# All six layer-2 tiles in pairs, with the weight sums made beside layer 1's last tile

## The reference

```
for t in range(768):                       # state per batch (4) and head (8), 48 x 48
    cur = einsum('bhd,bhe->bhde', u * k[t], v[t])
    y[t] = einsum('bhd,bhde->bhe', r[t], state + cur)
    state = w * state + einsum('bhd,bhe->bhde', k[t], v[t])
h = x @ w_in;  x = (h * sigmoid(1.702 * h)) @ w_out          # layer 1
h = x @ w_in2; out = (h * tanh(softplus(h))) @ w_out2        # layer 2
```

## Time and profile before

| | us |
|---|---|
| median of 3 runs | 878.36 |
| the profiled execution, its own time | 878.19 |
| its span, first to last instruction | 876.4 |
| PE busy | 869.5 |
| ACT busy | 345.1 |
| DVE busy | 330.9 |
| POOL busy | 216.6 |

### The profile page before, as it was taken

The page is one execution under the profiler, slowest core; times in us unless marked ns, Lnnn a source line. Parts: engine busy times, 40 slices in busy tenths (PEclk is TensorE's granted clock), DMA queues, the critical chain, the costliest instruction groups (busy, mean ns, idle before and its releaser), DMA issues.

```text
span 876.4 us, 13103 instructions
## 1 busy us (share of the span) xinstructions
PE 869.5 (99%) x5098; PEld 718.1 (82%) x5098; DVE 330.9 (38%) x501; ACT 345.1 (39%) x638; POOL 216.6 (25%) x200
## 2 busy tenths in 40 slices
PE   8999999999999999999999999999999999999998
PEld 7998888887888888778888888888888888888886
DVE  7756245424433442433254322211333333433333
ACT  4543232232223222322354532343544446544444
POOL 5869314222331432220000010173320003100000
PEclk9999999999999999999999999999999999999999
DMA  9454222312420422221431000110000000100001
GB/s 266 155 194 127 70 54 73 85 44 64 111 70 11 120 71 64 60 67 31 164 96 36 22 3 1 49 36 25 18 20 1 0 1 1 73 0 1 1 1 72
DMA packets 40432, 51.65 MB, mean 59 GB/s; under 512 B 6162, under 2 KB 32659, under 8 KB 40371
## 3 DMA queue, kind: packets, MB, share of 16 engines
q1 hardware_dynamic: 39840, 50.62, 19.8%
q10 hardware_dynamic: 530, 0.20, 0.1%
HBM read 38.21 MB, written 4.72 MB: 49 GB/s over the span
## 4 chain that ended last, share of the span: by engine, by line
PE 98%; DVE 1%; issue 0%; ACT 0%; POOL 0%; POOLq 0%; DVEq 0%; ACTq 0%
PE h L1352 31%; PE acc L1381 30%; PE h L1424 14%; PE acc L1520 7%; PE pair L1520 5%; PE a_bank L1231 3%; PE a_bank L1520 2%; PE pair L1264 2%; PE pair L1277 1%; PE a_bank L1289 1%; DVE wout_lo L1056 0%; PE pair L1214 0%; PE h L1231 0%; PE acc L1214 0%; DVE arena L1028 0%
## 5 line engine op out<-in xcount | busy, mean ns | idle before, releaser
L1352 PE MATMUL h<-xs,win_hi 128*128 128x512 f32 (+1 forms) x828 | 232.5, 380 | 0.9 <-DVE g_lo L1086 0.6
L1086 DVE TENSOR_TENSOR g_lo<-h,g_hi 128x512 fp32r<-128x512 f32 (+1 forms) x138 | 90.0, 652 | 332.1 <-ACT g_hi L767 332.1
L1352 PEld LDWEIGHTS h<-xs,win_hi 128*128 128x128 f32 x828 | 147.8, 188 | 31.2 <-issue 1.7
L763 ACT ACTIVATE h<-h 128x512 f32<-128x512 f32 (+1 forms) x138 | 76.2, 552 | 175.6 <-PE h L1352 172.7
L767 ACT ACTIVATE g_hi<-h 128x512 fp32r<-128x512 f32 (+1 forms) x138 | 78.3, 567 | 169.8 <-PE acc L1381 169.0
L1381 PE MATMUL acc<-g_hi,wout_hi 128*128 128x512 f32 (+1 forms) x414 | 112.6, 374 | 0.0
L1381 PE MATMUL acc<-g_hi,wout_lo 128*128 128x512 f32 (+1 forms) x414 | 112.4, 374 | 0.0
L1381 PE MATMUL acc<-g_lo,wout_hi 128*128 128x512 f32 (+1 forms) x414 | 112.4, 374 | 0.0
L1352 PE MATMUL h<-xs,win_lo 128*128 128x512 f32 (+1 forms) x414 | 110.4, 375 | 0.0
L577 POOL TENSOR_TENSOR arena<-arena 112x1024 f32<-112x1024 f32 x20 | 47.8, 2388 | 193.2 <-DMA arena<-in_rk 187.4
L1352 PEld LDWEIGHTS h<-xs,win_lo 128*128 128x128 f32 x414 | 75.0, 188 | 14.5
(11 more groups left out here) (154 smaller groups left out, 1117.1 us busy)
## 6 DMA issues: line engine op xcount, KB each, us to landing
arena<-in_rk SPq DMA_DIRECT2D x46, 192.0 KB, 3.4
mid<-in_wts SPq DMA_DIRECT2D x16, 384.0 KB, 7.3
arena<-in_wts SPq DMA_DIRECT2D x16, 384.0 KB, 3.4
xs<-xt SPq DMA_DIRECT2D x117, 48.0 KB, 2.0
arena<-in_k SPq DMA_DIRECT2D x22, 192.0 KB, 3.7
arena<-in_r SPq DMA_DIRECT2D x22, 192.0 KB, 4.0
arena<-in_v SPq DMA_DIRECT2D x22, 192.0 KB, 3.8
out<-mid SPq DMA_DIRECT2D x4, 768.0 KB, 3.3
```

The lines of the kernel that those rows point to most:

```text
L763: act.activation(h_cols(g), h_cols(g), GATES[layer]).then_inc(g_full, 1)
L1086: dve.tensor_tensor(g_lo[:, g % 2, cols], h_cols(g), f32(g_hi[:, g % 2, cols]), ALU.subtract).then_inc(glo_done, 1)
L1352: ins = pe.matmul(hb, w[:, f, kd, :], x_part(lo, par, kd)[:, c0:c1], start=i + kd == 0, stop=i == 2 and kd == KD - 1)
```

## The change

- Layer 2 has no plain tiles any more: TILES is 6 (layer 1 alone), PAIRS is 3. `split_mid` is gone, and `gate` serves layer 1 alone.
- The handover from tiles to quads now stands behind layer 1's last tile (tile 5), whose steps also split layer 2's weights.
- The weight sums are made from the staged weights in tile 5's steps, not from a reload. `stage` has four pieces: two in the area that later holds `h_sum`, `x_copy` and `seventh`, two in the place of tile 5's results in `mid`. A load into a piece waits for the low parts of the weight pair that used it too.
- The fourth weight sum is written over a raw block in its stage; its high and low parts always go to the place of feature block 0 of the odd hidden block, so odd w_in pieces are split for two of their three blocks.
- ScalarE does weight pair j in step 2j+2, the last in step 15; the table load moves to step 14. Factors B21 and B11 come in step 0, T2 and T3 in step 1, T4 in step 3, X20 in step 5.
- T4 and X20 change places in the order of factors, and `first_part` waits for X20 only ahead of its second product. The first pair's sums T2, T3, T4 lie in a free part of the arena, those of a later pair in the tile of `mid` before it.
- The split of w_out 15 goes into the first quad. The results of tile 5 are copied out when all weights are split.

```diff
-PLAIN = 2
-TILES = NT + PLAIN
-PAIRS = (NT - PLAIN) // 2
+TILES = NT
+PAIRS = NT // 2
-B21, B11, T2, T3, X20, T4, B22, X21, T1 = range(9)
+B21, B11, T2, T3, T4, X20, B22, X21, T1 = range(9)
...
-        STG = 8
-        stage = [arena[:, n * 2 * DM:(n + 1) * 2 * DM] for n in range(STG)]
+        shared = free(3 * TT, arena)
+        STG = 4
+        stage = [shared[:, 0:2 * DM], shared[:, 2 * DM:4 * DM]]
+        stage += [mid[:, (NT - 1) * KD * TT + n * 2 * DM:(NT - 1) * KD * TT + (n + 1) * 2 * DM] for n in range(2)]
...
         def raw_of(p, i):
-            t0 = PLAIN + 2 * p
+            t0 = 2 * p
             if i in (T2, T3, T4):
-                return mid_cols(0, (T2, T3, T4).index(i))
+                if p == 0:
+                    return t_first[:, 0:TT] if i == T2 else t_first[:, TT:2 * TT]
+                return mid_cols(t0 - 1, (T2, T3, T4).index(i))
...
         def fourth(j, lo):
-            return s4_more[:, lo] if j == FP - 1 else (win_hi, win_lo)[lo][:, 2 * j + 1, 0, :]
+            return (win_hi, win_lo)[lo][:, 2 * j + 1, 0, :]
...
 # SyncE, load_weights
                 if f >= STG:
                     sp.wait_ge(win_ready, NF + f - STG + 1)
                     sp.wait_ge(wout_ready, NF - 2 + f - STG + 1)
+                    sp.wait_ge(w_lo, 2 * ((f - STG) // 2 + 1))
...
 # GpSimd
             def weight_sums(j):
-                pool.wait_ge(w_raw_in[j % 2], 32 * (j // 2 + 1))
+                for f in (2 * j, 2 * j + 1):
+                    pool.wait_ge(stage_in[f % STG], 16 * (f // STG + 1))
                 if j:
                     pool.wait_ge(w_lo, 2 * j)
...
                 pool.wait_ge(w_sum, 4 * j + 3)
-                pool.tensor_tensor(w_sums[:, 3], raw[:, 0, 1], w_sums[:, 1], ALU.subtract).then_inc(w_sum, 1)
+                pool.wait_ge(win_ready, NF + 2 * j + 1)
+                pool.tensor_tensor(raw_in(j, 0, 1), raw_in(j, 0, 1), w_sums[:, 1], ALU.subtract).then_inc(w_sum, 1)
...
-            for i in (B21, B11):
-                factor_lo(0, i)
+            x_sums(0)
+            factor_lo(0, B21)
+            factor_lo(0, B11)
             weight_sums(0)
+            factor_lo(0, T2)
+            factor_lo(0, T3)
+            last_sum(0)
             for j in range(FP):
                 weight_lo(j)
                 if j + 1 < FP:
                     weight_sums(j + 1)
-                if j == 0:
-                    x_sums(0)
-                if j == 1:
-                    for i in (T2, T3, X20, T4):
-                        factor_lo(0, i)
+                if j < 2:
+                    factor_lo(0, (T4, X20)[j])
...
 # ScalarE
-            def tile(layer, par, t, last):
-                switch = layer == 0 and last
+            def tile(par, t, last):
                 for s, g in enumerate(range(BASE[t], BASE[t + 1])):
-                    if switch and g + 1 == BASE[t + 1]:
+                    if g + 1 < BASE[-1]:
+                        gate(g + 1)
+                    if g + 2 == BASE[-1]:
                         act.preload_act_table(GATES[1])
-                        gate(1, g + 1)
-                    elif g + 1 < BASE[-1]:
-                        gate(layer, g + 1)
...
-                    if switch:
+                    if last:
                         split_in(1, s)
                         if s >= 1:
                             split_out(1, s - 1)
...
+                        for i in {0: (B21, B11), 1: (T2, T3), 3: (T4,), 5: (X20,)}.get(s, ()):
+                            factor_hi(0, i)
+                        if s >= 2 and s % 2 == 0:
+                            weight_hi(s // 2 - 1)
+                        if s == NF - 1:
                             weight_hi(FP - 1)
...
             def quad(q):
                 if q == 0:
+                    split_out(1, NF - 1)
                     for i in (B22, X21, T1):
                         factor_hi(0, i)
...
 # TensorE
             def first_part(q):
                 j = q % FP
-                factors_there(q, X20 + 1)
+                if q < FP:
+                    pe.wait_ge(win_ready, NF + 2 * j + 2)
+                factors_there(q, B11 + 1)
...
                 product(x_bank, own(2 * j, 1), B21, True)
+                factors_there(q, X20 + 1)
                 product(x_bank, own(2 * j, 2), X20, False, True).then_inc(x_ready, 1)
```

More of the change, by code:

```diff
@@ L407, in mlp_rwkv_program, with run_tiles @@
         x_bank, sum_bank = h_bank[BASE[TILES] % 2], h_bank[(BASE[TILES] + 1) % 2]
[L409 to L412, removed]
+        def run_tiles(tile):
+            for t in range(TILES):
+                tile(t % 2, t, t == TILES - 1)
         @block.sync
@@ L507, in _ @@
                 load_weights(f)
[L509 to L526, removed]
             for p in range(PAIRS):
                 for i in range(2):
-                    t = PLAIN + 2 * p + i
+                    t = 2 * p + i
                     if t < NT - 2:
@@ L713, in _ @@
                 x_sums(p)
+                last_sum(p)
                 for i in range(FACTORS):
@@ L727, in split_in @@
                     raw = staged_in(f)
-                act.activation(win_hi[:, f], raw, ACT.Copy).then_inc(win_h, 1)
+                skip = layer and f % 2
+                act.activation(win_hi[:, f, skip:KD], raw[:, skip:KD], ACT.Copy).then_inc(win_h, 1)
             def split_out(layer, f):
@@ L767, in gate, with copy_out @@
                 act.activation(g_hi[:, g % 2, 0:c1 - c0], h_cols(g), ACT.Copy).then_inc(g_done, 1)
[L769 to L775, removed]
+            def copy_out(t, kds=BY_ACT):
+                layers = 2 if t == TILES - 1 else 1
+                act.wait_ge(win_ready, layers * NF)
+                act.wait_ge(wout_ready, layers * NF - 2)
+                if t == TILES - 1:
+                    act.wait_ge(w_lo, 2 * FP)
                 for kd in kds:
@@ L849, in tile @@
                             split_out(1, s - 1)
[L850 to L860 removed]
+                        for i in {0: (B21, B11), 1: (T2, T3), 3: (T4,), 5: (X20,)}.get(s, ()):
[3 more added lines that the diff above has]
+                        if s == NF - 1:
                             weight_hi(FP - 1)
[L862 to L863 removed]
+                if not last:
+                    copy_out(t)
             def weight_hi(j):
                 act.wait_ge(w_sum, 4 * (j + 1))
[L868 to L871 removed]
+                act.activation(s_hi[:, j], w_sums, ACT.Copy).then_inc(w_hi, 1)
+                act.wait_ge(h_done, BASE[TILES - 1] + 2 * j + 2)
+                act.activation(fourth(j, 0), stage[2 * j % STG][:, P:2 * P], ACT.Copy).then_inc(w_hi, 1)
             def factor_hi(p, i):
@@ L913, in pair_copy @@
             def pair_copy(p, i, kd):
-                act.wait_ge(f_lo, (p + 1) * FACTORS)
+                act.wait_ge(f_lo, (p + 1) * FACTORS + (T4 + 1 if i and p + 1 < PAIRS else 0))
                 if kd < KD - 1:
@@ L1140, in tile @@
                         decay_k(s // 7)
-                    if switch:
+                    if last:
                         split(s, s - 1 if s else None)
-                    if s == 1 and t == NT:
-                        split(None, NF - 1)
-                    if s in MID_STEPS and (layer == 1 and not last or switch):
-                        split_mid(1 - par, t + 1, MID_STEPS.index(s))
-                if t < TILES - 1:
-                    copy_out(layer, t)
+                if not last:
+                    copy_out(t)
             def pair_sum(n):
@@ L1189, in quad @@
                         pair_low(n + 1)
+                    if q == 0 and c == 0:
+                        split(None, NF - 1)
                     if q == 0 and c == 1:
-                        copy_out(1, TILES - 1)
+                        copy_out(TILES - 1)
                     if j == 0 and p and c < 2:
                         pair_copy(p - 1, c)
-            run_tiles(tile, 0)
-            run_tiles(tile, 1)
+            run_tiles(tile)
             for q in range(QUADS):
```

144 lines of the change are left out of this document (56 added, 88 removed).

## The result

The changed kernel took 879.67 us (median of 12 runs, 878.49 to 881.24), the kernel before 877.72 us beside it (12 runs, 877.25 to 878.95): a ratio of 1.0020, 95% interval 1.0011 to 1.0029. Measured once more in the first experiment, with runs of its own, the ratio was 1.0009 [0.9999, 1.0019]. The change buys nothing: by the first measurement it costs 2.0 us, by the second 0.8, which its interval does not tell from none.

A forecast was written before the change was run, and what follows sets the result against it. TensorE was taken to bound the kernel (busy 99%, 98% of the chain). From 878.36 us, -5.44 + 4.91 + 0.05 (one more split before the factors) + 0.8 = +0.3 gave 878.7 us; 8-in-10 range 877.0 to 882.3.

The forecast's parts named there:

- Matmuls removed: Layer 2's two plain tiles become a pair: 576 matmuls become 552, 24 fewer at 0.227 us, -5.44 us.
- The handover: From layer 1's last tile to the first quad: late weight results delay copy_x(0), so third(0) starts 4.9 us later.
- the lock: VectorE and GpSimd holding each other up when VectorE subtracts two SBUF tensors while GpSimd works; taken at +0.8 us.
- VectorE against GpSimd: In the handover's chain, two VectorE subtractions meet GpSimd's operations and one engine waits: +0.8 us, bounds 0 and 1.0.
- The upper bound: 1.0 us for VectorE and GpSimd contention, when each VectorE subtraction is let in between two GpSimd operations.
- The first rival: Slower: the idle gap before second(0) lowers TensorE's clock, +2.0 to +3.8 us, 880.7 to 882.5; chance 0.20.
- 21 matmuls, less 1.3 hidden: Upper clock price: second(0), third(0) and pair_down(0) all slow, +4.8 us, less 1.3 hidden in the second gap.
- Late loads: Layer 1's last tile: staging loads wait for weight sums with four stages; costed at nothing, 0 to 2 us each at worst.
- the order T4 then X20 at two boundaries: Pair boundaries: the second product waits for one more GpSimd operation, with 1.1 us of room; costed at nothing.
- The second rival: Slower: layer 1's last tile stalls on late loads or VectorE's queue, 879.5 to 882, most likely 880.7; chance 0.08.
- The rival on the other side: Faster: the last pair's weight results are done by 492.6, the handover's stall stays small, 872.9 us; chance 0.12.
- half way: The faster case with the handover's chain shorter by only 2 us: 876.5 us, sign turning from 1.5 us of shortening.

The follow-up runs named there:

- the first experiment: The changed kernel run again unaltered, beside the kernel before: 878.97 us against 878.22, ratio 1.0009.
- e4: Changed kernel with ScalarE's and VectorE's order in layer 1's last steps altered (sums 5 to 7 and w_in 14 earlier, table load last in step 14): 872.72 us.
- e6: Changed kernel with VectorE's subtractions for w_in 15 and w_out 14 moved from step 15 into the first quad: 879.45 us, ratio 1.0019.
- e2: Changed kernel with 16 spare matmuls on TensorE in the wait ahead of second(0): 878.45 us, ratio 0.9998.
- e5: Kernel before, with ten spare copies on ScalarE delaying copy_x(0): 884.43 us against 877.74, ratio 1.0076.
- e3: Changed kernel with the activation table load moved from step 14 to the end of step 15, behind the copy of sums 7: 877.36 us, ratio 0.9992.

## Why the prediction was right, point by point

The forecast was 878.7 us, "within 0.2%"; measured were 879.67 and, beside other runs, 878.97. As a difference from the kernel before, the forecast was +0.3 us, and +1.95 and +0.75 were measured. The starting value had luck in it: 878.36 was a median of three runs, 0.64 above that of twelve, and this brought the forecast nearer to the time that was measured.

- **Matmuls removed, -5.44.** Held. PE x5074, full windows in the quads, and e4 gets the whole of it.
- **The handover, +4.91.** Held. third(0) came 5.22 us later relative to first_part(0), of which 0.29 is the lock. Each link came at its length, from the table load to the 2.84 us (forecast 2.81) from the end of copy_x(0) to third(0).
- **VectorE against GpSimd, +0.8.** The mechanism was right, the size too large: 0.29 (e6). The upper bound had each of VectorE's two subtractions hold GpSimd up for its own 0.5 us. VectorE did most of the waiting (0.90 us for the one at 490.43, which takes 0.42 in e6's trace), and GpSimd lost only 0.18 and 0.11 us. The Trainium skill, SBUF — State Buffer, section Who interferes with whom, says that a VectorE instruction with two inputs in SBUF contends with a GpSimd instruction that reads SBUF. The rows agree (0.64 against 0.46 on GpSimd, 0.90 against 0.42 on VectorE); what it cost the chain was far less than the length of an operation.
- **The first rival, the clock.** I priced it as an alternative, and it came true together with the forecast. The Trainium skill, TensorE: Matmul & The Clock Gate, section HAM oscillation, says that idle gaps of TensorE can make the chip halve its clock. The trace agrees: a granted clock of 0.52 behind the gap. Its price was too high: 1.2 us (e2) instead of 2.0 to 3.8. The upper end was also added up wrongly: 4.8 less 1.3 is 3.5. The step that failed is "21 matmuls, less 1.3 hidden": the clock was back at 502.0, when third(0) ended, so pair_down(0)'s 9 matmuls never ran slowly. Of the 12 that did, six hid entirely in the second gap. In e5 the slow stretch lay later, nothing of it could hide, and it cost 2.6 us; which place it takes I could not have told from the profile of before.
- **Why the total fits.** In part by luck. The lock was 0.5 too dear and the clock, which the sum had at nothing, 1.2 too cheap: two errors of opposite sign. Of the sum of +0.3 the traces show +0.98 up to pair_down(0), and that is inside the forecast's own range. The rest of the 1.95 us between the first two medians, some 0.2 in the profiled span and what scatter adds, I didn't trace; the repeat gave 0.75.
- **Costed at nothing.** Late loads, VectorE's queue in the last tile, the order T4 then X20 at two boundaries: no wait of TensorE at any of them. The second rival didn't happen.
- **The rival on the other side** (weight results in time) didn't happen, but e4 shows that its arithmetic was right: 872.9 forecast for it, 872.72 measured once the order made it true. "Every link has a measured length" was the reason against it, and the links were only in that order because the kernel was written so. Two of its other figures don't follow from the sum: half way gives 878.7 - 2 = 876.7, not 876.5, and the sign of +0.3 turns with 0.3 us of shortening, not with 1.5.

## What to carry to other kernels

Before counting a saving on the bounding engine, follow the last result of the moved work through each queue it now stands in; if the order of three other engines was laid out for the old place, expect to need a new one, and here one that changed neither work nor buffers was worth 6 us. A new idle gap on TensorE can have a second price behind it: with 3.66 to 3.98 us in the profiles here the clock fell in nearly every run, with 2.91 in most. The price is smaller where the slow matmuls are followed by a wait for something else. A collision of two engines that exclude each other is worth looking up by who waits: here most of it fell on the one that wasn't on the chain.

## What the runs showed of the hardware

TensorE's granted clock fell to about half for a few microseconds after a gap in one place of a run that is otherwise full. With a gap of 3.98 us the whole run's clock was under 0.999 in all 23 runs of the changed kernel, with 3.68 us in nine of the ten of e6, with 3.66 us in all four of e5, with 2.91 in 7 of 10 (e3), and with 0.44 us or the gap filled in none. The gaps are those of the profiled run of each kernel; those of the other runs are not known. When it falls isn't fixed: the changed kernel's clock was already low when second(0) began, in e5 it fell some 1.4 us after second(0) had begun, and the cost behind the gap differed accordingly. In both profiled runs the slow stretch was some 7 us, an estimate from the windows (0.82 over the 4.1 us of the gap, if it is a step from 1.0 to 0.5, is a fall at about 495.1, and the clock is full again from 502.0; in e5, 0.67 over 2.5 us and 0.64 over the last 3 make it from about 628.3 to 635.2). It is not as long in every run: 8 of the 23 have a whole run's clock of 0.998 and not 0.996 or 0.997, which is 3 to 4 us at half the clock. For the first of these, the windows of the changed kernel over the last matmuls of layer 1 and over the gap:

```profile
486.40:492.50 6.10, 6.10 (x28) 4.88 (x26) 3.35 (x5) 4.16 (x8) 2.30 (x4) 1.00 0.00 0
492.50:496.60 4.10, 0.20 (x1) 0.00 (x0) 0.00 (x0) 1.32 (x3) 2.57 (x5) 0.82 0.00 0
```

Why it comes earlier in the one than in the other stays open; no run was made to tell that.
